# Attention beside the second layer of the first dense expert, two pairs of heads at a time

## The reference

```python
# attention: batch 2, 8 heads, 576 positions, head_dim 64, window 64
scores = scale * np.matmul(q, k.transpose(0, 1, 3, 2))
mask = (rel >= 0) & (rel < window)
scores = np.where(mask, scores, -1000000000.0)
scores = scores - np.max(scores, axis=-1, keepdims=True)
attn = np.exp(scores)
attn = attn / (np.sum(attn, axis=-1, keepdims=True) + 1e-09)
return np.matmul(attn, v).astype(np.float32)
...
# dense experts: N = 1152 rows, D = 512, E = 4, F = 1024
for e in range(E):
    h = np.maximum(x @ w1[e], 0.0)
    out += p[:, e:e + 1] * (h @ w2[e])
...
# routed experts: E = 8, each row goes to one expert or none
h = np.maximum(xc[mask] @ w1[e], 0.0)
y[mask] = gate_w[mask, None] * (h @ w2[e])
```

## Time and profile before

| what | us |
|---|---|
| median of 3 runs (range) | 631.36 (630.97 to 631.39) |
| profiled execution, its own time | 630.76 |
| its span | 629.2 |
| TensorE busy | 616.4 (98%) |
| VectorE busy | 292.0 (46%) |
| ScalarE busy | 245.1 (39%) |
| GpSimd busy | 75.3 (12%) |

### The profile page before, as it was taken

One profiled execution on the slowest core, in us unless ns is written; L12 is line 12 of the kernel. 1 busy time (PEld: TensorE's weight loads), 2 busy tenths in 40 slices (PEclk: granted clock), 3 DMA queues, 4 the chain that ended last, 5 costly groups with the idle time before them and its releaser, 6 DMA issues.

```text
span 629.2 us, 9696 instructions
## 1 busy us (share of the span) xinstructions
PE 616.4 (98%) x3433; PEld 550.0 (87%) x3434; DVE 292.0 (46%) x760; ACT 245.1 (39%) x520; POOL 75.3 (12%) x121
## 2 busy tenths in 40 slices
PE   7999999999999999999999999999999999999995
PEld 6889999898989898989999998989888888888884
DVE  5576556524512124412124332354567744771681
ACT  5765546422401013301103121222335764863771
POOL 6660000000000000000000000010111311221221
PEclk9999999999999999999999999999999999999999
DMA  8744134007999995210001231042467857693541
GB/s 283 221 124 120 54 99 136 35 1 224 233 240 234 257 257 180 75 61 0 0 0 66 73 128 51 18 136 87 178 241 270 275 147 245 220 355 68 168 157 22
DMA packets 51314, 90.27 MB, mean 143 GB/s; under 512 B 13128, under 2 KB 17736, under 8 KB 51280
## 3 DMA queue, kind: packets, MB, share of 16 engines
q1 hardware_dynamic: 47088, 82.15, 43.4%
q0 software_dynamic: 3520, 7.53, 4.8%
q10 hardware_dynamic: 672, 0.15, 0.1%
HBM read 64.15 MB, written 27.08 MB: 145 GB/s over the span
## 4 chain that ended last, share of the span: by engine, by line
PE 96%; DVE 1%; ACT 1%; DMA 1%; issue 1%; POOL 0%; SPq 0%; DVEq 0%; POOLq 0%; ACTq 0%
PE ps_y L1181 31%; PE ps_h L1181 31%; PE ps_y L1270 11%; PE ps_h L1270 10%; PE ps_s L1079 2%; PE ps_o L1124 2%; PE ps_s L1285 2%; PE ps_s L1158 1%; PE ps_t L1094 1%; PE ps_h L1205 1%; PE ps_t L1259 1%; DMA qz<-q 1%; PE ps_t L1146 1%; ACT prob L635 0%; PE ps_h L1067 0%
## 5 line engine op out<-in xcount | busy, mean ns | idle before, releaser
L708 ACT ACTIVATE ht_hi<-ps_h 128x384 fp32r<-128x384 f32 (+1 forms) x104 | 48.6, 467 | 238.4 <-PE ps_h L1181 231.5
L1181 PE MATMUL ps_h<-xt_hi,w_hi_a 128*128 128x384 f32 (+1 forms) x400 | 130.7, 327 | 0.0
L1181 PE MATMUL ps_h<-xt_hi,w_lo_a 128*128 128x384 f32 (+1 forms) x400 | 129.4, 324 | 0.0
L1181 PE MATMUL ps_h<-xt_lo,w_hi_a 128*128 128x384 f32 (+1 forms) x400 | 129.3, 323 | 0.0
L1181 PE MATMUL ps_y<-w_hi_a,ht_hi 128*128 128x512 f32 x288 | 114.6, 398 | 0.0
L1181 PE MATMUL ps_y<-w_hi_a,ht_lo 128*128 128x512 f32 x288 | 112.6, 391 | 0.0
L1181 PE MATMUL ps_y<-w_lo_a,ht_hi 128*128 128x512 f32 x288 | 112.4, 390 | 0.0
L939 DVE SCALAR_TENSOR_TENSOR ht_lo<-ps_h,ht_hi 128x384 fp32r<-128x384 f32 (+1 forms) x104 | 54.7, 526 | 119.1 <-ACT ht_hi L708 118.9
L1181 PEld LDWEIGHTS ps_h<-xt_hi,w_hi_a 128*128 128x128 f32 x400 | 75.3, 188 | 0.5 <-DVE ht_lo L939 0.2
L1181 PEld LDWEIGHTS ps_h<-xt_lo,w_hi_a 128*128 128x128 f32 x400 | 75.4, 188 | 0.3
L1181 PEld LDWEIGHTS ps_h<-xt_hi,w_lo_a 128*128 128x128 f32 x400 | 75.3, 188 | 0.0
(11 more groups left out here) (176 smaller groups left out, 829.7 us busy)
## 6 DMA issues: line engine op xcount, KB each, us to landing
raw<-u SPq DMA_DIRECT2D x36, 512.0 KB, 4.8
x_sorted<-xg SPq DMA_DIRECT2D x4, 4112.0 KB, 44.6
raw<-w SPq DMA_DIRECT2D x32, 512.0 KB, 4.3
x<-u SPq DMA_DIRECT2D x24, 512.0 KB, 5.6
vt<-v SPq DMA_DIRECT2D x17, 256.0 KB, 2.9
xg<-x_sorted POOLq DMA_DIRECT2D x13, 257.0 KB, 5.2
kt<-k SPq DMA_DIRECT2D x8, 384.0 KB, 4.5
x_sorted<-xg SPq DMA_DIRECT2D x1, 2313.0 KB, 44.4
```

What stands on the lines that cost most here:

```text
L708: a.activation(ht_hi[:, pos, 0:P * tiles], ps_h[:, pos % 2, 0:P * tiles], ACT.Relu).then_inc(h_hi_done, 1)
L1181: ins = mm(dst, hi_lo[l], rhs_hi_lo[r], start=(first and n == 0), stop=(last and n == 2))
```

## The change

`attention` stays for the prologue. For pairs 8 to 35 there is a new unit, a *group* of two pairs: group g does the scores of pairs 2g and 2g+1, the transposes of pairs 2g-2 and 2g-1 (four, side by side in `ps_t`, copied by one copy of 512 columns), and PV of pairs 2g-4 and 2g-3. Groups 4 to 9 stand in chunk 0, 10 to 13 in chunk 1, 14 to 19 in chunk 2, all after positions of the second layer; groups 18 and 19 have no scores, group 19 no transposes. Counted from the first position of the second layer, they stand after positions 0, 2, 5, 7, 10 and 12, in chunk 1 after 0, 3, 7 and 11. VectorE's part is cut in two: `group` at that position (masks of both pairs, normalising of the first), `group_end` one position later (normalising of the second, `xt_lo` of the group before last). In the prologue odd pairs transpose into a bank of `ps_y` instead of `ps_t` (`turned_probs`), so that a transpose waits for the copy of two pairs ago, not of the last; `xt_lo` of pair 3 stands one step later; the first fill has 11 matmuls instead of 9, and two later fills move. Keys come already cut into tiles of 192 columns, so that a load is one contiguous piece for each partition.

```diff
@@ -85,20 +85,28 @@
         return PAIRS * tiles + LAG + 1
     PROLOGUE = steps_for(FIRST_CHUNKS[0][1])
-    FILL_FIRST, FILL = 9, 1
+    def groups_for(tiles):
+        return PAIRS * tiles // 2 + 2
+    GROUPS = PAIRS * NT // 2
+    FIRST_GROUP = PAIRS * FIRST_CHUNKS[0][1] // 2
+    FILL_FIRST, FILL = 11, 1
     PROLOGUE_PIECES = [1, 2, 4, 5]
     def beside_first(c):
         at = weight_pieces(c, True)
         if c < len(FIRST_CHUNKS) - 1:
-            begin, end = (steps_for(sum(FIRST_CHUNKS[i])) for i in (c, c + 1))
-            room = FC + FIRST_CHUNKS[c][1] * FC - 1
-            steps = [("attention", p) for p in range(begin, end)]
+            begin, end = (groups_for(sum(FIRST_CHUNKS[i])) for i in (c, c + 1))
+            room = FIRST_CHUNKS[c][1] * FC - 1
             if c == 0:
-                steps = [("scores", p) for p in range(begin - LAG - 1, begin)] + steps
-            for n, step in enumerate(steps):
-                at.setdefault(n * room // len(steps), []).append(step)
+                begin = FIRST_GROUP
+            for n, g in enumerate(range(begin, end)):
+                pos = FC + n * room // (end - begin)
+                at.setdefault(pos, []).append(("group", g))
+                at.setdefault(pos + 1, []).append(("group_end", g))
         return at
@@ -297,6 +305,11 @@
             return ps_y[:, 0, :] if r < EARLY and r // 2 % 2 else ps_o[:]
+        def turned_probs(r):
+            bank = ps_y[:, 1, :] if r < EARLY and r % 2 else ps_t[:]
+            return bank[:, 0:HALVES * P]
         def compact_outputs(xt, r):
@@ -358,12 +371,11 @@
                 if t >= 3:
                     sp.wait_ge(scores_ready, PAIRS * (t - 2))
-                b, n0 = t % 3, P * t
+                b = t % 3
                 for j in range(2):
                     load_queries(sp, t, j)
-                lo = max(0, n0 - WINDOW)
-                sp.dma_start(kt[:, b, :, lo - (n0 - WINDOW):KEYS],
-                             k[:, lo:n0 + P].rearrange("(a p) n -> p a n", p=P)).then_inc(keys_landed[b], 16)
+                sp.dma_start(kt[:, b].rearrange("p a n -> p (a n)"),
+                             k[:, t].rearrange("p a n -> p (a n)")).then_inc(keys_landed[b], 16)
             def load_values(t):
@@ -375,8 +387,7 @@
                     lo = max(0, n0)
                     sp.dma_start(vt[lo - n0:P, t % 2, half, :], v[lo:n0 + P, :]).then_inc(values_landed[t % 2], 16)
-            sp.dma_start(kt[:, 0, :, WINDOW:KEYS],
-                         k[:, 0:P].rearrange("(a p) n -> p a n", p=P)).then_inc(keys_landed[0], 16)
+            sp.dma_start(kt[:, 0, :, WINDOW:KEYS], k[:, 0, :, WINDOW:KEYS]).then_inc(keys_landed[0], 16)
             load_queries(sp, 0, 0)
             load_values(0)
             load_keys(1)
@@ -634,15 +645,30 @@
                     own = prob[:, u % BUFFERS, :]
                     a.activation(own, own, ACT.Exp, bias=least[:, u % BUFFERS:u % BUFFERS + 1], scale=-1.0,
                                  accum_out=sums[:, u % BUFFERS:u % BUFFERS + 1]).then_inc(probs_ready, 1)
-                if p == PROLOGUE - 1:
-                    copy_probs(EARLY)
             def copy_probs(r):
                 act.wait_ge(pt_ready, r + 1)
                 if r >= 2:
                     act.wait_ge(pv_done, r - 1)
-                copy(prob_t[:, r % 2].rearrange("p s n -> p (s n)"), ps_t[:, 0:HALVES * P]).then_inc(pt_copied, 1)
+                copy(prob_t[:, r % 2].rearrange("p s n -> p (s n)"), turned_probs(r)).then_inc(pt_copied, 1)
+            def group(g):
+                if g < GROUPS:
+                    scores(2 * g)
+                if FIRST_GROUP <= g - 1 < GROUPS:
+                    act.wait_ge(pt_ready, 2 * g)
+                    act.wait_ge(pv_done, 2 * g - 2)
+                    copy(prob_t[:].rearrange("p r s n -> p (r s n)"), ps_t[:]).then_inc(pt_copied, 2)
+                if g < GROUPS:
+                    scores(2 * g + 1)
+                if FIRST_GROUP <= g - 2:
+                    act.wait_ge(pv_done, 2 * g - 2)
+                    for j in range(2):
+                        dst, src = outputs(xt_hi, 2 * g - 3, j)
+                        copy(dst, src).then_inc(xt_hi_done, 1)
             def first_half(j):
...
@@ -844,10 +870,21 @@
                         d.tensor_scalar(prob[:, u, :], prob[:, u, :], sums[:, u:u + 1], None,
                                         ALU.mult).then_inc(probs_normal, 1)
-            def scores(p):
-                mask_scores(p)
-                if p > EARLY:
-                    normalise(p - 1)
+            def group(g):
+                if g < GROUPS:
+                    mask_scores(2 * g)
+                    mask_scores(2 * g + 1)
+                    normalise(2 * g)
+            def group_end(g):
+                if g < GROUPS:
+                    normalise(2 * g + 1)
+                if FIRST_GROUP <= g - 2:
+                    for j in range(2):
+                        dve.wait_ge(xt_hi_done, 2 * g - 3 + j)
+                        dst, src = outputs(xt_lo, 2 * g - 3, j)
+                        minus_hi(dst, src, outputs(xt_hi, 2 * g - 3, j)[0]).then_inc(xt_split, 1)
             def attention(p):
                 if p < EARLY or PROLOGUE <= p < NPAIR:
@@ -855,7 +892,12 @@
                 r = p - 1
                 if 0 <= r < EARLY or PROLOGUE - 1 <= r < NPAIR:
                     normalise(r)
-                if p < PROLOGUE - 1:
+                if p == EARLY - 1:
+                    r = -1
+                elif p == EARLY:
+                    r = p - LAG - 3
+                elif p < PROLOGUE - 1:
                     r = p - LAG - 2
                 else:
                     r = p - LAG - 1
...
@@ -1080,24 +1124,25 @@
                               qz[:, t % 3, a, half].rearrange("p j n -> p (j n)"),
                               kt[:, t % 3, a, WINDOW * half:WINDOW * half + P], start=True, stop=True)
                 last.then_inc(scores_ready, 1)
-                if p == PROLOGUE - 1:
-                    turn_probs(EARLY)
             def turn_probs(r):
                 if r == 0:
                     pe.wait_ge(masks_made, 2)
                 pe.wait_ge(probs_normal, 2 * r + 2)
-                if r >= 1:
+                if 2 <= r < EARLY:
+                    pe.wait_ge(pt_copied, r - 1)
+                elif r >= EARLY:
                     pe.wait_ge(pt_copied, r)
                 for half in range(HALVES):
-                    last = turn(ps_t[:, P * half:P * half + P], prob[:, (2 * r + half) % BUFFERS, :], ident[:])
+                    last = turn(turned_probs(r)[:, P * half:P * half + P], prob[:, (2 * r + half) % BUFFERS, :], ident[:])
                 last.then_inc(pt_ready, 1)
             def attention(p):
                 if p < EARLY or PROLOGUE <= p < NPAIR:
                     scores(p)
-                if p < PROLOGUE:
+                if p <= EARLY:
                     fill(FILL)
                 r = p - LAG
                 if 0 <= r < EARLY or PROLOGUE - LAG <= r < NPAIR:
@@ -1124,6 +1169,35 @@
                             last = mm(output_bank(r)[:, P * (2 * (r % 2) + half):P * (2 * (r % 2) + half) + P],
                                       vt[:, t % 2, half, P * a:P * a + P], prob_t[:, r % 2, half, :], start=True, stop=True)
                     last.then_inc(pv_done, 1)
+                if p == EARLY + 1:
+                    fill(FILL)
+            def group(g):
+                if g < GROUPS:
+                    scores(2 * g)
+                    scores(2 * g + 1)
+                if FIRST_GROUP <= g - 1 < GROUPS:
+                    pe.wait_ge(probs_normal, 4 * g)
+                    pe.wait_ge(pt_copied, 2 * g - 2)
+                    for i in range(2):
+                        for half in range(HALVES):
+                            n0 = P * (2 * i + half)
+                            last = turn(ps_t[:, n0:n0 + P], prob[:, (4 * g - 4 + 2 * i + half) % BUFFERS, :], ident[:])
+                        last.then_inc(pt_ready, 1)
+                if FIRST_GROUP <= g - 2:
+                    t = (2 * g - 4) // PAIRS
+                    pe.wait_ge(pt_copied, 2 * g - 2)
+                    pe.wait_ge(values_landed[t % 2], 16 * 2 * (t // 2 + 1))
+                    pe.wait_ge(xt_split, 2 * g - 4)
+                    for r in (2 * g - 4, 2 * g - 3):
+                        a = r % PAIRS
+                        for half in range(HALVES):
+                            n0 = P * (2 * (r % 2) + half)
+                            last = mm(ps_o[:, n0:n0 + P], vt[:, t % 2, half, P * a:P * a + P], prob_t[:, r % 2, half, :],
+                                      start=True, stop=True)
+                        last.then_inc(pv_done, 1)
             def route(stage, t):
                 if stage == "turn" and t == NT - 1:
...
@@ -1364,9 +1436,12 @@
     B, H, S, HD = q.shape
     N = B * S
     E1, E2 = moe_w1.shape[0], moe2_w1.shape[0]
+    window = P // 2
```

(20 more changed lines are left out.)

## The result

The changed kernel takes 639.56 us (median of 4 runs, 638.24 to 639.81), the kernel before 631.30 beside it (4 runs, 630.97 to 631.39): a ratio of 1.0126, interval 1.0114 to 1.0139. It is slower by 8.3 us, where 5.4 were forecast. The profiled execution took 639.68 us with a span of 638.1, 8.92 more than that of before.

The account below looks back on a forecast made before the run. TensorE, busy 98%, bounds the kernel. Stalls of 8.8 against 2.75 now, less 0.3 for switches, give +5.75; prologue -0.4, keys 0: +5.35 on 630.76 is 636.1, by median 636.7 us; range 632.2 to 640.

Parts of the forecast that it names:

- rival C: In GpSimd's shadow, VectorE operations block fully: 2.5 us more at group 5, 0.5 at group 6, 639.7; chance 9%.
- The ring: Second-layer groups: PV, copy, second pair's exps, normalising, xt_lo, next PV take 4.39 us; stall 0.81 at gap two, 0.12 at three.
- x update: VectorE's x update of 0.75 us falls into group 7 and adds 0.2; also counted in the wait at group 18.
- rivals A: The second layer hides the groups: waits from PV to PV close within 3.6 us, no stall left, 627.8 by median; 12%.
- B: Waits from PV to PV close at 3.9 us, normalising fast at group 5: stalls about 4, 631.8 to 633.8; 12%.
- Group 5's stall: Chunk 0, group 5's transposes wait for two normalisings slowed by GpSimd, 1.78 us each: 2.35 us, bounds 0.55 and 2.97.
- Rival D: No attention stall at group 5, since GpSimd runs earlier: 1.8 us less, 634.9; chance 12%.
- What a stall costs: TensorE's stalls beside the first expert, each counted at its own length: 8.8 us after the change, 2.75 before.
- Block 4 and the end of chunk 0: First-layer block 4 waits 0.33 us for w1_lo's second half; at chunk 0's end TensorE waits 0.35 for xt_lo.
- fewer switches: 31 attention insertions become 16, saving TensorE 0.3 us; a group takes 2.20 against 2 x 1.11 for two steps.
- The prologue: Two transpose banks, earlier normalising and a moved fill save 0.55 us, two added fills cost 0.15: -0.4, bounds -1.2 and +0.2.
- The keys: Loading keys as whole tiles, same bytes: 0 us; at best 0.72 less, at worst 0.

Follow-up runs that it names:

- Experiment 1: Changed kernel with ScalarE doing the exps of both pairs of a group ahead of the copy of transposed probabilities: 634.75 us, ratio 1.0050.
- experiment 3: Changed kernel with 11 filler matmuls between the scores and the transposes of group 5: 637.45 us, ratio 1.0098.
- experiment 2: Changed kernel with pairs 8 to 11 normalised in the prologue's form, inverse sums in PSUM and one product: 635.38 us, ratio 1.0066.
- experiment 4: Kernel before with only the rearranged prologue and the keys in tiles, attention still in single steps: 631.02 us, ratio 0.9995.
- experiment 8: Changed kernel with 9 fillers instead of 11 ahead of the first scores: 638.94 us, ratio 1.0119.
- experiment 7: Changed kernel with its groups spread over both layers of a chunk instead of the second only: 632.99 us, ratio 1.0029.

## Why the prediction was right, and where its size was off

The sign, the place and the mechanism of the stalls held; the forecast was 2.9 us short. That the result lies inside the range, 0.4 us under its upper end, is in part luck: it lies above the 638.5 that the forecast gave for itself, and the range reached to 640 for rival C, whose mechanism did not occur (its 639.7 meets the 639.56 only by chance).

**The ring: right, but for the x update.** 4.39 worked out, 4.38 and 4.46 measured; a gap of two lost 0.83 to 0.85 (0.81), a gap of three 0.16 (0.12, and 0.32 at group 8 with the x update). The copy came 0.15 later after PV than taken, the normalising was 0.07 shorter. The x update of VectorE, taken to add 0.2 to the ring after group 7 and at group 18, added nothing that the trace shows: it ends at 53.34, and the normalising starts 0.90 after the exps (52.41 to 53.31), as it does without an update (47.95 to 48.85). Experiment 1 shows the cause of the ring; rivals A (3.6 us) and B (3.9) fall by its length. The sum over chunk 1 and chunk 2 is 4.0 (3.8): 0.16 in chunk 1, then 0.83, 0.16, 0.85, 1.07 at group 18 (121.59 to 126.05 is 4.46, TensorE's own 3.39) and 0.90 at group 19 (3.16 against 2.26).

**Group 5's stall: right in kind, 0.5 short.** 2.35 forecast, 2.86 measured. The mis-sized term is the normalising in GpSimd's shadow, taken as 1.78, the mean of three in the trace of before, of which one had a slow first operation. Both of those that count here had it, and took 1.95 and 2.04, 0.43 more in all; TensorE was also 0.06 earlier at the transposes (3.16 after group 4's scores, not 3.22); the upper bound in the prediction, 2.97, was with both at 2.09. Rival C, three whole subtractions held up per normalising, would have needed 3.1 each and falls. Rival D falls too: GpSimd did start earlier (29.56, 7.4 after the dense start instead of 8.3), but its subtractions ran until 40.68, past both normalisings.

**What a stall costs: the step that failed.** The prediction priced each stall at its own length. Behind the 2.69 us of idleness TensorE's granted clock fell to 0.50, and nine records took 1.58 more. The term was missing from the sum and from every rival, and experiment 3 shows it. With it two normalisings that are 1.1 and 1.2 us longer than in the other form cost 3.65 us (experiment 2).

**Block 4 and the end of chunk 0.** 0.33 forecast, 0.41 measured; 0.35 forecast, 0.45 measured.

**The sum.** 0.41 + 2.86 + 1.58 + (0.83 + 0.16 + 0.85 + 0.45) + 0.16 + 3.81 = 11.1 us of loss against 8.8 forecast. Less the 2.75 of before it is 8.4, and the stretch grew by 8.42. The 0.3 that the prediction took off for fewer switches is not there: a group that meets no wait takes 2.14 us (44.96 to 47.10) and 0.09 more in the first dense record after it (47.10 to 47.42 against 0.23), together 2.23, where two steps take 2 x 1.11 = 2.22; and without their stalls the two stretches are alike, 110.12 - 11.1 = 99.0 and 101.70 - 2.75 = 98.95.

**The prologue: too hopeful.** -0.4 forecast, -0.06 in the profile and nothing in experiment 4. The wait ahead of the last xt_hi is as long as before (ScalarE idles 1.27 us there, 1.22 before). The 0.15 for two more fills was also wrong: they lie in the wait for q.

**The keys:** 0, as forecast.

## What to carry to other kernels

Work out a ring of waits over all engines' queues (here PV, copy, exps, normalising, xt_lo, PV) and hold it against TensorE's own work in the gap: an operation that nothing in the ring needs early should still stand ahead of one that waits. Price a stall of TensorE of some microseconds above its length, look at the granted clock behind it, and fill it where it can't be removed. Merging steps makes each wait hold up more work (here a chain of 4.4 us against 3.6 of work in the gap), so positions must be chosen anew.

## What was not expected of the hardware

- After idling 2.69 us TensorE's granted clock was 0.50 for about 3 us, with TensorE busy throughout; after 2.88 in experiment 1 the same, and after 2.69 again in experiment 8. It fell only when TensorE was busy again, some 0.7 us after the idle time had ended (at about 41.5), in experiment 1 1.4 after it (at about 43.0). With idle times up to 0.64 in experiment 2, and with the stall filled, it stayed at 1.00.
- A TENSOR_SCALAR on 128x2 elements takes 0.17 us alone, and beside GpSimd's subtractions (11.12 us for 16, so 0.70 each) 0.60 and 0.70 at group 5 and 0.74 in experiment 7: held up by over half of one, while the reciprocal of the same shape stays at 0.17. Not each is held up so long: three beside them in the kernel before took 0.25, 0.19 and 0.73 (at 31.71, 35.25 and 38.18 us). What decides it was not tried.
- The first 22 fills take 5.06 us from 1.30 on, the same 22 in experiment 3 take 2.62 at 37.67; the granted clock reads 1.00 in both stretches. In experiment 4's profile the first 22 take 4.65. Why the first are at about half the rate is open.

```profile
1.30 5.06 PE L1111 MATMUL ps_h<-xr 128*128 128x128 f32 x22 [1.30 <-DVE xr L1058]
```
